# Turning gathered rows with VectorE, in squares of 32, in the down phases of a mixture-of-experts kernel

## The chip, the core and the metric

The kernel runs on one core of a Trainium2 chip. The core has TensorE (PE in the profile, with its weight loads as PEld), VectorE (DVE), ScalarE (ACT), GpSimd (POOL) and SyncE (SP); each works through a queue of its own in order, and they wait for each other by semaphores. The metric is the time of one execution in device microseconds, and the median of three is given.

## What is computed

Three layers follow each other: windowed attention, a gated dense layer, and a mixture of eight experts with two chosen per row. The change lies in the last one.

```python
def _moe2_ref(x, w_gate, w_noise, noise, w1, w2):        # x (2304, 512), w1 (8, 512, 1024), w2 (8, 1024, 512)
    ...                                                 # the two best experts of each row and their weights
    for e in range(E):
        for k in range(2):
            mask = top2[:, k] == e
            ...
            h = np.maximum(x[mask] @ w1[e], 0.0)
            out[mask] += top2_w[mask, k, None] * (h @ w2[e])
```

## The kernel before

**Tiles.** Each expert is given five tiles of 128 rows (`TILES` = 5; `HEAD` = 3 tiles make the first part, `LATE` = 2 the second). GpSimd gathers the 128 rows of tile n from memory into one of two buffers, `x_g[:, n % 2]`, by an indirect DMA (`gather`, L588). The rows lie across the partitions then, and the up product wants the 512 columns across them, in four blocks of 128, so each tile is turned: TensorE does it in `turn_g(n)` (L816), four transposes of 128 x 128 (L822) into one bank, `ps_xt`. ScalarE's `xt_high(n)` (L1066) rounds the turned tile to the format of the products, VectorE's `xt_low(n)` (L1364) takes the remainder; the two halves stand in `xT[p]`. Weights are split in the same manner: eight units per expert arrive in four buffers `raw`, ScalarE's `high(e, n)` (L1052) and VectorE's `low(e, n)` (L1350) make the two halves, and SP loads the next unit when `low` has read its buffer (`load_expert`, L421).

**Order of an expert.** `up(e, p, f)` (L825) multiplies part p with block f of w1 (12 matmuls, 384 columns wide for p = 0 and 256 for p = 1) into one of two banks; ScalarE's `relu` and VectorE's `hidden_low` (L1370) empty it into `hT`. Block f may start when `hidden_low` of block f - 2 is done. After 16 blocks comes the down phase: `down(e, a)` (L842) multiplies the hidden rows of tile a with w2 (24 matmuls of 512 columns), ScalarE's `rows_out` (L1087) scales the result, and GpSimd's `scatter` (L591) adds it to the output in memory, by an indirect DMA.

**Where the turning stands.** Nothing schedules this: each engine's order is written out in its own function. In the down phase of expert e, the five tiles of expert e + 1 are turned, one behind each `down(e, a)`. ScalarE's queue reads there: `high(e+1, a)` for a < 4, `rows_out(e, a)`, `xt_high` of the tile; VectorE's: `low(e+1, a)` for a < 4, `xt_low` of the tile. In the next up half the queues read `relu`, `high` of a unit of w2, and `hidden_low`, `low` of it, for the first four blocks. The first 15 tiles are turned at other places: 0 to 9 in the end of the dense layer and in expert 0, tile 10 behind the last down of expert 0, 11 and 12 inside the second up half of expert 1, 13 and 14 behind its first two downs. `gather(n)` waits until tile n - 2 has been turned (`xt_turned`), and its place in GpSimd's queue is behind `scatter(n - 7)` from tile 17 on.

The index e runs from 0 to 7 everywhere; the last expert's down phase turns nothing. Rows beyond the five tiles of an expert are handled by `left_tile` in a loop that runs as often as such tiles are left.

Of the kernel before, what the change touches and what calls it, by code (L numbers as in the profile page):

```python
# [13 lines left out]
P = 128  # L14


def attention_two_moe_program(nc, q, k, v, gv, w_out, r_gate, r_noise, noise, w1, w2, out):
# [12 lines left out]
    KC = DM // P  # L30
# [31 lines left out]
    PER = TT  # L62
    COLS = NE * PER
# [11 lines left out]
    with ExitStack() as ctx:  # L75
# [64 lines left out]
        more_i = sb("more_i", [P, 3, MORE], I32)  # L140
        idx_r = sb("idx_r", [P, 1], I32)
# [160 lines left out]
        ORDER = [0, 1, 2, 5, 6, 7, 3, 4, 8, 9] + list(range(AHEAD * TILES, ALL))  # L302

# [203 lines left out]
        def _(pool):  # L507
# [137 lines left out]
            for n in (12, 13, 14):  # L645
                gather(n)
            scatter(5)
            gather(15)
            scatter(6)
            gather(16)  # L650
            for m in (7, 8, 9):
                scatter(m)
            for m in range(AHEAD * TILES, ALL):
                scatter(m)
                if m + 7 < ALL:
                    gather(m + 7)
# [20 lines left out]
        def _(pe):  # L677
# [251 lines left out]
            turn_g(10)  # L929
            for f in range(F2C):  # L930
                up(1, 1, f)
                if f in (2, 5):
                    turn_g(11 + f // 3)
            for a in range(TILES):
                down(1, a)
                if a < 2:
                    turn_g(13 + a)
            for e in range(AHEAD, NE):
                for p in range(2):
                    for f in range(F2C):  # L940
                        up(e, p, f)
                for a in range(TILES):
                    down(e, a)
                    if e < NE - 1:
                        turn_g(TILES * (e + 1) + a)
# [27 lines left out]
        def _(act):  # L973
# [92 lines left out]
            def xt_high(n):  # L1066
                e, a = divmod(ORDER[n], TILES)
                p, cols = part(a)
                act.wait_ge(xt_turned, n + 1)
                if e:  # L1070
                    act.wait_ge(up_done, F2C * (half_no(e - 1, p) + 1))
                elif p == 0:
                    act.wait_ge(gv_done, LAST - FC + 6)
                else:
                    act.wait_ge(hr_used, LAST)
                act.copy(xT[p][:, 0, :, cols], ps_xt.rearrange("p (k m) -> p k m", k=KC)).then_inc(xt_hi, 1)  # L1076
# [98 lines left out]
            xt_high(10)  # L1175
            for f in range(F2C):
                relu(1, 1, f)
                if f < KC:
                    high(1, KC + f)
                if f in (2, 5):  # L1180
                    xt_high(11 + f // 3)
            for a in range(TILES):
                if a < KC:
                    high(AHEAD, a)
                rows_out(1, a)
                if a < 2:
                    xt_high(13 + a)
# [31 lines left out]
        def _(dve):  # L1219
# [143 lines left out]

            def xt_low(n):  # L1364
                p, cols = part(ORDER[n] % TILES)
                dve.wait_ge(xt_hi, n + 1)
                dve.tensor_tensor(xT[p][:, 1, :, cols], ps_xt.rearrange("p (k m) -> p k m", k=KC),  # L1367
                                  xT[p][:, 0, :, cols].bitcast(F32), ALU.subtract).then_inc(xt_lo, 1)
# [117 lines left out]
            xt_low(10)  # L1486
            for f in range(F2C):
# [3 lines left out]
                if f in (2, 5):  # L1491
                    xt_low(11 + f // 3)
            for a in range(TILES):
                if a < KC:
                    low(AHEAD, a)
                if a < 2:
                    xt_low(13 + a)
            for e in range(AHEAD, NE):
# [5 lines left out]
                for a in range(TILES):  # L1504
                    if e < NE - 1 and a < KC:
                        low(e + 1, a)
# [42 lines left out]
```

## Time and profile before

| | before |
|---|---|
| median of 3 runs (lowest to highest) | 1055.52 us (1055.36 to 1055.85) |
| the profiled execution, its span from first to last instruction | 1058.44 us, 1056.8 us |
| TensorE busy | 1029.5 us, 97% of the span |
| VectorE, ScalarE, GpSimd busy | 392.2, 387.8, 234.5 us |
| mean granted clock of TensorE | 0.986 |
| memory traffic | 95.28 MB, 90 GB/s on average |

The profile comes from one execution, which took longer than the median of the runs. Busy time says how long an engine had an instruction in work; matmuls overlap, so a busy TensorE is not one at its peak. The granted clock is the share of 2.4 GHz that the chip allowed TensorE: 1.0 is that, 0.5 is 1.2 GHz.

### The profile page before, as it was taken

The numbers are of one execution on the slowest core, as the hardware profiler recorded it, in microseconds if no ns is written. First come the engines' busy times: TensorE is split into PE (matmuls) and PEld (weight loads), VectorE is DVE, ScalarE is ACT, GpSimd is POOL, SyncE is SP. The second block draws the span as 40 slices with busy tenths as digits, with TensorE's granted clock in tenths as the row PEclk, the third lists the DMA queues.
The fourth block names the chain that finished last, engine by engine and source line by source line (L and its number), as shares of the span: only waits on it lengthen the run. The fifth ranks groups of instructions, "written<-read, shape, count | busy, mean of one in ns | idle before, by whom it ended". The sixth has DMA issues, their size and how long they took to land. (4 is left out here: it accounts for less than half of the span.)

```text
span 1056.8 us, 18749 instructions
## 1 busy us (share of the span) xinstructions
PE 1029.5 (97%) x7455; PEld 940.8 (89%) x7455; DVE 392.2 (37%) x1113; ACT 387.8 (37%) x941; POOL 234.5 (22%) x225
## 2 busy tenths in 40 slices
PE   6999999999999999999999999999999999999994
PEld 5999999999999999999999898799898989898983
DVE  3662343342434334242345434433432424343310
ACT  4553243433424333342344433333333333333310
POOL 2581022021111202111022322211304030312111
PEclk6999999999999999999999999999999999999998
DMA  5662113121211212110224232662616263543312
GB/s 174 205 196 71 31 46 96 52 75 51 81 51 50 62 51 81 51 51 1 100 81 147 69 101 41 184 155 58 163 59 153 88 159 100 140 120 100 60 14 37
DMA packets 48249, 95.28 MB, mean 90 GB/s; under 512 B 9504, under 2 KB 14624, under 8 KB 48160
## 3 DMA queue, kind: packets, MB, share of 16 engines
q1 hardware_dynamic: 35696, 66.22, 19.0%
q0 software_dynamic: 12032, 27.31, 12.7%
q8 instruction: 61, 1.00, 0.4%
q10 hardware_dynamic: 432, 0.52, 0.2%
q14 instruction: 28, 0.23, 0.1%
HBM read 72.35 MB, written 21.68 MB: 89 GB/s over the span
## 5 line engine op out<-in xcount | busy, mean ns | idle before, releaser
L760 PEld LDWEIGHTS bank<-xr,wr 128*128 128x128 f32 x2592 | 326.5, 191 | 9.4 <-issue 0.5
L760 PE MATMUL bank<-xr,wr 128*128 128x256 f32 x2592 | 329.3, 283 | 0.0
L838 PE MATMUL bank<-wr 128*128 128x256 f32 (+1 forms) x1536 | 229.8, 310 | 0.6 <-DVE xr L1373 0.3
L838 PEld LDWEIGHTS bank<-wr 128*128 128x128 f32 x1536 | 226.1, 190 | 1.4 <-DVE wr L1373 0.6
L777 PE MATMUL bank<-wr,hr 128*128 128x512 f32 x648 | 176.5, 407 | 0.0
L1267 DVE SCALAR_TENSOR_TENSOR arena<-arena,bank 128x256 f32<-128x256 f32 x108 | 45.4, 420 | 253.0 <-ACT arena L1015 253.0
L1015 ACT ACTIVATE arena<-bank 128x256 f32<-128x256 f32 x108 | 41.5, 384 | 265.9 <-PE bank L760 265.8
L853 PE MATMUL bank<-wr 128*128 128x512 f32 x576 | 136.3, 393 | 0.0
L777 PEld LDWEIGHTS bank<-wr,hr 128*128 128x128 f32 x648 | 113.7, 188 | 23.2 <-issue 2.2
L853 PEld LDWEIGHTS bank<-wr 128*128 128x128 f32 x576 | 106.6, 188 | 21.5
L601 POOL DMA_INDIRECT out<-arena,tab x34 | 53.4, 1572 | 283.8 <-ACT arena L1094 275.3
L529 POOL TENSOR_TENSOR arena<-arena 128x512 f32<-128x512 f32 (+1 forms) x32 | 32.2, 1006 | 319.3 <-DVE arena L1242 319.3
L853 PE MATMUL bank<-wr,xr 128*128 128x512 f32 x384 | 90.8, 393 | 0.0
L1362 DVE TENSOR_TENSOR wr<-arena,wr 128x1024 fp32r<-128x1024 f32 x64 | 78.1, 1225 | 26.6 <-ACT wr L1064 26.6
L853 PEld LDWEIGHTS bank<-wr,xr 128*128 128x128 f32 x384 | 71.2, 188 | 14.4
L1273 DVE TENSOR_TENSOR hr<-arena,hr 128x256 fp32r<-128x256 f32 x108 | 64.4, 596 | 48.2 <-ACT hr L1022 48.2
L1094 ACT ACTIVATE arena<-bank,tab 128x512 f32<-128x512 f32 x34 | 23.4, 690 | 144.1 <-PE bank L853 144.1
L1367 DVE TENSOR_TENSOR wr<-bank,wr 128x512 fp32r<-128x512 f32 x40 | 27.6, 691 | 127.4 <-ACT wr L1076 127.2
L1064 ACT CAST wr<-arena 128x1024 fp32r<-128x1024 f32 x64 | 66.7, 1047 | 0.0
L1022 ACT CAST hr<-arena 128x256 fp32r<-128x256 f32 x108 | 43.9, 406 | 59.0 <-DVE arena L1267 59.0
L571 POOL DMA_INDIRECT places<-pairs,slot_i x36 | 36.2, 1006 | 115.0 <-DVE pairs L1348 106.7
L1373 DVE SCALAR_TENSOR_TENSOR wr<-bank,wr 128x384 fp32r<-128x384 f32 x64 | 35.7, 557 | 64.8 <-ACT wr L1085 64.7
(121 smaller groups left out, 781.5 us busy)
## 6 DMA issues: line engine op xcount, KB each, us to landing
arena<-moe_w SPq DMA_DIRECT2D x64, 512.0 KB, 4.4
arena<-gv SPq DMA_DIRECT2D x12, 512.0 KB, 3.8
out<-zeros POOLq DMA_DIRECT2D x20, 256.0 KB, 2.7
arena<-v SPq DMA_DIRECT2D x18, 256.0 KB, 2.7
x_rows<-arena SPq DMA_DIRECT2D x9, 512.0 KB, 3.1
arena<-v SPq DMA_DIRECT2D x34, 128.0 KB, 2.7
arena<-k SPq DMA_DIRECT2D x17, 256.0 KB, 3.5
arena<-q SPq DMA_DIRECT2D x16, 256.0 KB, 3.6
```

The costliest lines, as they stand in the source:

```text
L571: pool.indirect_dma_start(places[:, :], bass.IndirectOffsetOnAxis(slot_i[:, t, c:c + 1], 0), pairs[:, t, c], None).then_inc(placed if g < ...
L601: pool.indirect_dma_start(out[:, :], bass.IndirectOffsetOnAxis(row_no(m), 0), y_s[:, m % 2], None, compute_op=ALU.add).then_inc(scattered[ ...
L760: mm = pe.matmul(o, gv_w[:, f, w, kk], xr[:, g % 2, x, kk], start=(m + kk + n == 0), stop=(kk == KC - 1 and n == 2), skip_group_check=True)
L777: mm = pe.matmul(ps_y[t], hr[:, f % 2, a, t * P:(t + 1) * P], wo_w[:, b, f], start=(f == 0 and n == 0), stop=(f == FC - 1 and n == 2))
L838: mm = pe.matmul(ps_h[u % 2][:, 0:n], w1_r[e % 2][:, a, kk, f * P:(f + 1) * P], xT[p][:, b, kk], start=(kk + x == 0), stop=(kk == KC - 1 a ...
L853: mm = pe.matmul(ps_e[m % 2], hT[p][:, i, f, cols], w2_r[:, j, f], start=(f + x == 0), stop=(f == F2C - 1 and x == 2))
L1015: act.activation(gate[:, r], ps_g[r][:, 0:GT], ACT.Tanh, scale=0.5).then_inc(gate_done, 1)
L1022: act.copy(hr[:, r, 0], gate[:, r]).then_inc(h_hi, 1)
L1064: act.copy(unit(e, n, 0), raw[:, n % 4]).then_inc(e_hi, 1)
L1267: dve.scalar_tensor_tensor(out=gate[:, r], in0=gate[:, r], scalar=1.0, in1=ps_g[r][:, GT:2 * GT], op0=ALU.add, op1=ALU.mult).then_inc(h_do ...
L1273: dve.tensor_tensor(hr[:, r, 1], gate[:, r], hr[:, r, 0].bitcast(F32), ALU.subtract).then_inc(h_lo, 1)
L1362: dve.tensor_tensor(unit(e, n, 1), raw[:, n % 4], unit(e, n, 0).bitcast(F32), ALU.subtract).then_inc(e_lo, 1)
```

## The change

From tile 10 on (`SQUARES` = `AHEAD * TILES`), TensorE turns no tile. VectorE does it in `turn_rows(n)`: 16 transposes of a square of 32 x 32 in each of the four column blocks, so of 32 partitions by 128 elements, from `x_g` into a new tensor `x_t` of 128 x 4 x 128 in on-chip memory. `xt_high` and `xt_low` read `x_t` in place of the bank (`turned_at`). `turn_rows` waits for the gather, and for `xt_high` and `xt_low` of the tile before, since `x_t` is single. It stands at the head of each tile's work in VectorE's queue in the down phase. The tiles of expert 2 (10 to 14) move into expert 1's down phase, as those of the later experts are in the phase before theirs, and GpSimd's gathers from tile 12 on all stand behind a scatter.

```diff
+    SQUARES = AHEAD * TILES
+    Q4 = P // 4
...
+        x_t = sb("x_t", [P, KC, P])
...
+        def turned_at(n):
+
+            return ps_xt.rearrange("p (k m) -> p k m", k=KC) if n < SQUARES else x_t[:]
...
@@ gpsimd
-            for n in (12, 13, 14):
-                gather(n)
-            scatter(5)
-            gather(15)
-            scatter(6)
-            gather(16)
-            for m in (7, 8, 9):
-                scatter(m)
-            for m in range(AHEAD * TILES, ALL):
+            for m in range(TILES, ALL):
                 scatter(m)
                 if m + 7 < ALL:
                     gather(m + 7)
@@ tensor
             down(0, 4)
-            turn_g(10)
             for f in range(F2C):
                 up(1, 1, f)
-                if f in (2, 5):
-                    turn_g(11 + f // 3)
             for a in range(TILES):
                 down(1, a)
-                if a < 2:
-                    turn_g(13 + a)
...
                 for a in range(TILES):
                     down(e, a)
-                    if e < NE - 1:
-                        turn_g(TILES * (e + 1) + a)
@@ scalar
-                act.copy(xT[p][:, 0, :, cols], ps_xt.rearrange("p (k m) -> p k m", k=KC)).then_inc(xt_hi, 1)
+                act.copy(xT[p][:, 0, :, cols], turned_at(n)).then_inc(xt_hi, 1)
...
             for a in range(TILES):
                 if a < KC:
                     high(AHEAD, a)
                 rows_out(1, a)
-                if a < 2:
-                    xt_high(13 + a)
+                xt_high(SQUARES + a)
@@ vector
+            def turn_rows(n):
+                dve.wait_ge(gathered[n % 2], 16 * (n // 2 + 1))
+                if n > SQUARES:
+                    dve.wait_ge(xt_hi, n)
+                    dve.wait_ge(xt_lo, n)
+                dve.nop(nofuse=True)
+                rows = x_g[:, n % 2].rearrange("p (k m) -> p k m", k=KC)
+                for b in range(4):
+                    at = slice(b * Q4, (b + 1) * Q4)
+                    for a in range(4):
+                        to = slice(a * Q4, (a + 1) * Q4)
+                        tr = dve.transpose(x_t[to, :, at], rows[at, :, to])
+                tr.then_inc(xt_turned, 1)
...
             for a in range(TILES):
+                turn_rows(SQUARES + a)
                 if a < KC:
                     low(AHEAD, a)
-                if a < 2:
-                    xt_low(13 + a)
+                xt_low(SQUARES + a)
...
                 for a in range(TILES):
+                    if e < NE - 1:
+                        turn_rows(TILES * (e + 1) + a)
                     if e < NE - 1 and a < KC:
                         low(e + 1, a)
                     if e < NE - 1:
                         xt_low(TILES * (e + 1) + a)
```

VectorE's queue at the end of a down phase with turning and the start of the next up half, before. L1362 is `low` (behind `up_done` of a w1 unit, behind `down_done` of a w2 unit), L1367 `xt_low`, L1373 `hidden_low`:

```order
L1362 TENSOR_TENSOR wr<-arena,wr 128x1024 [waits up_done,e_hi]
L1367 TENSOR_TENSOR wr<-bank,wr 128x4x128 [waits xt_hi]
L1362 TENSOR_TENSOR wr<-arena,wr 128x1024 [waits up_done,e_hi]
L1367 TENSOR_TENSOR wr<-bank,wr 128x4x128 [waits xt_hi] x2
L1373 SCALAR_TENSOR_TENSOR wr<-bank,wr 128x384 [waits ht_hi]
L1362 TENSOR_TENSOR wr<-arena,wr 128x1024 [waits down_done,e_hi]
```

And the same place in the changed kernel, where L1364 is the squares, L1351 `low`, L1370 `xt_low` and L1376 `hidden_low`:

```order
L1364 STREAM_TRANSPOSE x_t<-arena 32x4x32 [waits xt_lo,gathered0,xt_hi]
L1364 STREAM_TRANSPOSE x_t<-arena 32x4x32 x15
L1351 TENSOR_TENSOR wr<-arena,wr 128x1024 [waits up_done,e_hi]
L1370 TENSOR_TENSOR wr<-x_t,wr 128x4x128 [waits xt_hi]
L1364 STREAM_TRANSPOSE x_t<-arena 32x4x32 [waits xt_lo,gathered1,xt_hi]
L1364 STREAM_TRANSPOSE x_t<-arena 32x4x32 x15
L1370 TENSOR_TENSOR wr<-x_t,wr 128x4x128 [waits xt_hi]
L1376 SCALAR_TENSOR_TENSOR wr<-bank,wr 128x384 [waits ht_hi]
L1351 TENSOR_TENSOR wr<-arena,wr 128x1024 [waits down_done,e_hi]
```

The last two tiles of the phase are shown: 16 squares now stand ahead of each `low` or `xt_low`, and the first hidden row of the next expert stands behind those of the fifth tile.

TensorE's queue between the last tile of a down phase (L853) and the next up half (L838), before and then changed; L822 is the turn:

```order
L853 MATMUL bank<-wr,xr 128x512 [waits ht_lo]
L853 MATMUL bank<-wr,xr 128x512 x2
L822 MATMUL bank<-ident,arena 128x128 [waits gathered1,xt_lo]
L822 MATMUL bank<-ident,arena 128x128 x3
L838 MATMUL bank<-wr 128x384 [waits ht_lo,e_lo,xt_lo]
L838 MATMUL bank<-wr 128x384 x11
L838 MATMUL bank<-wr 128x384 [waits ht_lo]
```

```order
L853 MATMUL bank<-wr,xr 128x512 [waits ht_lo]
L853 MATMUL bank<-wr,xr 128x512 x2
L838 MATMUL bank<-wr 128x384 [waits ht_lo,e_lo,xt_lo]
L838 MATMUL bank<-wr 128x384 x11
L838 MATMUL bank<-wr 128x384 [waits ht_lo]
```

The turn, with its wait for the gather, is gone, and the up half follows the last tile at once.

## Rows read from the trace of the kernel before

**Rows 1.** The page, part 1: busy us, share of the span, instructions.

```profile
PE 1029.5 (97%) x7455; PEld 940.8 (89%) x7455; DVE 392.2 (37%) x1113; ACT 387.8 (37%) x941; POOL 234.5 (22%) x225
```

**Rows 2.** TensorE's waits: who waited for whom, us in total, times, longest.

```profile
PE bank L822 <- DMA arena<-x_rows,tab: 1.7, 1, 1.7
```

**Rows 3.** Timeline, TensorE, down phase of expert 3: start, length, instructions, [idle before].

```profile
783.65 5.64 PE L853 MATMUL bank<-wr 128*128 128x512 f32 x24
...
813.18 28.41 PE L838 MATMUL bank<-wr 128*128 128x384 f32 x192
```

**Rows 4.** Timeline, TensorE, down phase of the last expert.

```profile
1014.75 16.51 PE L853 MATMUL bank<-wr 128*128 128x512 f32 x72
1031.09 11.04 PE L853 MATMUL bank<-wr,xr 128*128 128x512 f32 x48
```

**Rows 5.** Timeline, TensorE, second up half of expert 1.

```profile
654.51 4.55 PE L838 MATMUL bank<-wr 128*128 128x256 f32 x36
...
658.89 0.60 PE L822 MATMUL bank<-ident,arena 128*128 128x128 f32 x4
...
669.49 5.63 PE L853 MATMUL bank<-wr 128*128 128x512 f32 x24
```

**Rows 6.** Timeline, all engines, down phase of expert 2.

```profile
725.87 5.63 PE L853 MATMUL bank<-wr 128*128 128x512 f32 x24
...
726.49 0.42 DVE L1373 SCALAR_TENSOR_TENSOR xr<-bank,xr 128x256 fp32r<-128x256 f32 x1 [1.02 <-ACT xr L1085]
...
737.48 0.69 ACT L1094 ACTIVATE arena<-bank,tab 128x512 f32<-128x512 f32 x1 [3.83 <-PE bank L853]
...
738.93 1.57 POOL L601 DMA_INDIRECT out<-arena,tab  x1 [2.98 <-ACT arena L1094]
739.63 1.23 DVE L1362 TENSOR_TENSOR wr<-arena,wr 128x1024 fp32r<-128x1024 f32 x1 [0.26 <-ACT wr L1064]
740.81 1.01 POOL L588 DMA_INDIRECT arena<-x_rows,tab  x1 [0.30 <-issue]
```

**Rows 7.** Timeline, first blocks of the up half of expert 3.

```profile
755.83 0.58 ACT L1076 CAST wr<-bank 128x512 fp32r<-128x512 f32 x1
756.44 0.69 DVE L1367 TENSOR_TENSOR wr<-bank,wr 128x512 fp32r<-128x512 f32 x1 [5.22 <-ACT wr L1076]
...
757.78 0.49 ACT L1085 ACTIVATE wr<-bank 128x384 fp32r<-128x384 f32 x1 [1.38 <-PE bank L838]
...
758.30 0.56 DVE L1373 SCALAR_TENSOR_TENSOR wr<-bank,wr 128x384 fp32r<-128x384 f32 x1 [1.18 <-ACT wr L1085]
...
759.86 0.49 ACT L1085 ACTIVATE wr<-bank 128x384 fp32r<-128x384 f32 x1 [0.65 <-PE bank L838]
```

**Rows 8.** Timeline, VectorE, attention: masked scores, no wait between.

```profile
12.10 0.29 DVE L1231 CUSTOM_DVE_ANT_0 arena<-bank,mask 128x128 f32<-128x128 f32 x1 [2.45 <-PE bank L706]
...
12.32 0.28 DVE L1231 CUSTOM_DVE_ANT_0 arena<-bank,mask 128x128 f32<-128x128 f32 x1
```

**Rows 9.** Timeline, VectorE: two instructions, the second awaiting the first.

```profile
643.00 0.27 DVE L1467 TENSOR_TENSOR arena<-arena 128x104 f32<-128x104 f32 x1
643.30 0.26 DVE L1468 TENSOR_REDUCE arena<-arena 128x8 f32<-128x104 f32 x1
```

**Rows 10.** DMA issues: count and median us from issue to landing, gathers.

```profile
arena<-x_rows,tab POOLq DMA_INDIRECT x34, 5.1
```

**Rows 11.** Timeline, TensorE, the opening.

```profile
9.80 1.03 PE L724 MATMUL bank<-ident,arena 128*64 128x128 f32 x4 [2.74 <-DVE arena L1248]
```

**Rows 12.** Stretches: busy us of PE, PEld, DVE, ACT, POOL; clock, DMA, GB/s.

```profile
9.00:10.00 1.00, 0.20 (x2) 0.20 (x3) 0.60 (x2) 1.00 (x6) 0.00 (x0) 0.86 1.05 414
...
25.00:26.00 1.00, 1.00 (x22) 0.88 (x22) 0.00 (x0) 0.28 (x2) 0.00 (x0) 0.50 0.98 328
...
30.00:31.00 1.00, 1.00 (x10) 1.00 (x9) 0.00 (x0) 0.00 (x0) 0.00 (x0) 0.90 0.98 318
```

**Rows 13.** The same view, around the wait for tile 12.

```profile
664.00:668.00 4.00, 2.26 (x20) 2.08 (x19) 1.11 (x3) 0.97 (x2) 0.47 (x1) 1.00 0.98 383
```

More of the change, by code:

```diff
@@ L1174, in _ @@
             rows_out(0, 4)
-            xt_high(10)
             for f in range(F2C):
@@ L1179, in _ @@
                     high(1, KC + f)
-                if f in (2, 5):
-                    xt_high(11 + f // 3)
             for a in range(TILES):
@@ L1366, in xt_low @@
                 dve.wait_ge(xt_hi, n + 1)
-                dve.tensor_tensor(xT[p][:, 1, :, cols], ps_xt.rearrange("p (k m) -> p k m", k=KC),
+                dve.tensor_tensor(xT[p][:, 1, :, cols], turned_at(n),
                                   xT[p][:, 0, :, cols].bitcast(F32), ALU.subtract).then_inc(xt_lo, 1)
@@ L1485, in _ @@
             xt_low(9)
-            xt_low(10)
             for f in range(F2C):
@@ L1490, in _ @@
                     low(1, KC + f)
-                if f in (2, 5):
-                    xt_low(11 + f // 3)
             for a in range(TILES):
+                turn_rows(SQUARES + a)
                 if a < KC:
                     low(AHEAD, a)
-                if a < 2:
-                    xt_low(13 + a)
+                xt_low(SQUARES + a)
             for e in range(AHEAD, NE):
```

## The prediction

> **What bounds the kernel now.** I read the page's busy times first. TensorE is busy for 97% of the span and VectorE for 37% [rows 1], so a step that is cut from TensorE's queue shows in the end time, and VectorE has room on average. The waits of TensorE come next: behind the opening, the longest is 1.7 us, the turn of tile 12 waiting for its gathered rows [rows 2]. The end of the kernel is therefore the sum of TensorE's own work. What has to be read after that is one down phase, because the change puts new work on VectorE only there: the average of 37% does not say whether five tiles of turning fit beside five tiles of multiplying.
>
> **What the change removes from TensorE.** 30 turns of four matmuls go: tile 10 behind the first expert, 11 to 14 around the second, and five in each down phase of experts 2 to 6 (numbered from 0). In expert 3 the down phase with its five turns takes 813.18 - 783.65 = 29.53 us [rows 3]. The last expert has no turns: three tiles take 1031.09 - 1014.75 = 16.34 us, 5.45 us each and 27.24 for five [rows 4]. So 2.29 us go per down phase, 0.46 per turn, and 5 x 2.29 = 11.5 us for experts 2 to 6. In expert 1, the second up half holds turns 11 and 12 and the 1.7 us wait. It takes 669.49 - 654.51 = 14.98 us; 36 of its matmuls take 658.89 - 654.51 = 4.38 us, so 96 take 11.68 [rows 5]. That is 3.3 us. Turns 10, 13 and 14 add 3 x 0.46 = 1.4. In all **16.2 us** are taken off TensorE. The last expert's tiles follow each other without a gap, so I expect none between the tiles where the turns stood.
>
> **What it adds on VectorE.** 16 square instructions per tile, each 32 partitions by 128 elements, 480 in all. No row shows a square, nor an instruction that reads or writes other partitions than the one before it. I bound the time from one start to the next by two kinds of rows. Instructions that may overlap: one of 128 elements and its accumulator read start again after 0.21 us, though the first is 0.29 us long [rows 8]. Instructions that each await the one before: 104 elements, start to start 0.30 us, 0.27 us long [rows 9]; 24 more elements at about 1 ns make 0.29 us of length and 0.32 from start to start. So a tile costs between 16 x 0.21 = 3.4 us and 16 x 0.32 = 5.2 us. I take **0.31 us and 4.96 us per tile**. The reason is where they start: in the overlapping rows one instruction follows another on the same 128 lanes, while each square writes another group of 32 partitions than the last (and every fourth reads another), so I place it nearer to the rows that run one after the other; 0.31 is the length of such an instruction with a little of the gap.
>
> The Trainium skill has a rule on this (VectorE: DVE Perf Modes, section on two Vector instructions with no wait between them): an instruction that starts in another quadrant of 32 partitions than the last read or write of that memory is held until all earlier ones have finished. By it all 16 squares are held, which is against this change, and no row here shows it. The same page's section on the three transpose paths gives 311 ns for 128 x 128 elements of 2 bytes; an estimate with it is 16 x 0.311 = 4.98 us per tile, and the total would be the same as mine, while squares that overlapped would make the whole change free, as below.
>
> **Whether that fits.** I count from the start of a down phase, where TensorE would start tiles at 0, 5.45, 10.9, 16.3, 21.8 and the next up half at 27.24. VectorE is free at 1.1: its last hidden row starts 0.62 after the phase and is 0.42 long [rows 6]. Its queue is now, per tile, squares, then the low part of a weight unit (1.23 us) [rows 6], then the low part of the tile (0.69) [rows 7], with 0.1 of overlap and as much of semaphores, 1.9 us in all. The squares of the next tile wait for that last one, because x_t is a single buffer. So the fifth tile is turned at 1.1 + 5 x 4.96 + 4 x 1.9 = 33.5. ScalarE's high part (0.58), VectorE's low part (0.69) and then VectorE's first hidden row of the next expert (0.56) [rows 7] stand behind it in both queues, with some 0.1 of semaphores: 35.5. TensorE may start the third block of the up half only after that hidden row, since the two banks alternate. It would be there at 27.24 + 2 x 2.08 = 31.4 (blocks go by in 2.08 us: 759.86 - 757.78 [rows 7]). **TensorE waits 4.1 us.** There are six such phases (experts 1 to 6), so 24.6 us. The first blocks of the up half need tile 3 of 5 turned (about 20.5) and the fourth weight unit's low part (1.1 + 4 x 4.96 + 3 x 1.9 + 1.2 = 27.9), 0.6 late, which lies inside the same wait. After the third block VectorE needs 0.56 + 1.23 = 1.8 us per block against 2.08, so the delay isn't repeated.
>
> **What else moves.** GpSimd gathers tile n+2 behind the scatter of one tile of the same phase. A scatter starts 1.5 us and a gather 3.3 us after ScalarE starts that tile's output [rows 6], and a gather lands 5.1 us after its issue [rows 10]: 3.0 us after the next tile ends. The squares would start for it at the earliest at that point or, by the chain above, later, so it costs nothing at 4.96 us per tile; and at 3.4 us per tile the 1 us it adds is within the room there. ScalarE now waits with the high part of a tile for the squares, and the next output of rows stands behind that: the first four tiles are turned at 6.1, 12.9, 19.8 and 26.7, the outputs behind them are due at 10.9, 16.3, 21.8 and 27.24, so outputs and scatters keep their times and TensorE finds its banks free. The high part reads on-chip memory in place of a bank; 0.1 us more would add 0.6 to the total. SP's loads of units 4 to 7 wait for the low parts of units 0 to 3; the last is asked for at 27.9 and needed by ScalarE behind the fourth block, after 37, and the nearest landing time, 5.1 us [rows 10], fits. GpSimd's gathers of tiles 12 to 16 now stand behind scatters 5 to 9, as those of the later phases do, and no longer make TensorE wait. What is priced at nothing here would be seen as a wait if the squares were short; behind a wait of 4.1 us it is covered.
>
> **The clock.** A wait of 4 us may cost more than itself. After a wait of 2.74 us of TensorE in the opening, behind sparse work, the clock went from 1.0 to 0.5 (from 2.4 to 1.2 GHz) at about 9.9 us, and came back at about 30, with TensorE busy without a break from 25 on: some 4.5 us [rows 11, 12]. With 1.74 us of wait inside full work it stayed at 1.0 [rows 13]. So each fall costs about half of 4.5, 2.2 us. I count it for three of the six phases, **6.6 us**; bounds 0 and 6 x 2.2 = 13.
>
> **The sum.** -16.2 + 24.6 + 6.6 = +15.0 us. The profiled execution took 1058.44 us (span 1056.8), 2.9 over the median of 1055.52; the median is the one forecast: 1055.5 + 15.0 = **1070.5 us**, and a profile of it some 1073.
>
> **Rivals.**
> A, the squares overlap. At 0.21 us per square a tile costs 3.4 us, the fifth tile is turned at about 28.5 (bounded by TensorE's tiles, no longer by VectorE), the hidden row is ready at 30.4, before 31.4. No wait, the whole gain stays: 1055.5 - 16.2 = 1039.3. For it: VectorE does overlap neighbours in the trace. Against it: the squares change partitions. The point from which it turns is a wait of more than zero at 0.25 us per square, and break-even (16.2 / 6 = 2.7 us of wait) at about 0.29. Chance 0.15.
> B, the squares are a little shorter than I take them, 0.27 to 0.29 us: waits of 1.5 to 2.6 us, no fall of the clock, 1048 to 1056. Each ns per square is 80 ns per phase, half a us on the total. Chance 0.12.
> C, the forecast: 0.30 to 0.325 us, waits of 3.3 to 5.2 us, 1058.9 to 1070.9 without the clock, up to 13 more with it. Chance 0.5.
> D, the squares are longer (a fill of the square before it empties): 0.34 us make 6.4 us of wait per phase and a fall in each: 1055.5 - 16.2 + 38.7 + 13 = 1091. Chance 0.18; of still longer ones, above 1092, 0.05.
>
> **Numbers.** C is the likeliest and gives 1070.5. A range from 1046 to 1092 leaves out A and the very long squares, 2 in 10. Faster by over 0.2% (2.1 us, about what a measurement of this kernel can tell): A and two thirds of B, 0.22. Within 0.2%: 0.04. Slower: 0.74.
>
> **What the profile would show.** The step on TensorE is right if down phases take 27.2 us without a matmul of L822's kind among them. The price is right if squares start 0.31 us apart and the fifth tile's last one ends about 33.5 us after the phase starts. The wait is right if TensorE's longest waits are six of about 4 us on the hidden low rows, at the third block of an up half. Wrong would be: squares 0.2 us apart (A); a wait at the first block instead of the third (the weight unit's low part); or waits on gathered rows.

## The result and the profile after

| | before | changed |
|---|---|---|
| median (lowest to highest) of 4 runs | 1055.65 us (1055.36 to 1055.85) | 1083.01 us (1081.05 to 1084.53) |
| ratio, 95% interval | | 1.0257 (1.0241 to 1.0274) |
| span of the profiled execution | 1056.8 us | 1082.8 us |
| mean granted clock | 0.986 | 0.973 |

The change makes the kernel 27.4 us slower; the two spans differ by 26.0. The page of the changed kernel, busy us, share of the span and instructions, to be held against [rows 1]:

```profile
PE 1029.8 (95%) x7335; PEld 939.7 (87%) x7335; DVE 536.3 (50%) x1593; ACT 389.3 (36%) x941; POOL 243.3 (22%) x225
```

TensorE has 120 transposes less and no less busy time, although they were worth 15 us (experiment 3): something else grew. VectorE went from 392 to 536 us, half of the span. That still looks like an engine with room, and it is the wrong number to look at. TensorE's waits, who waited for whom, us in total, times, longest:

```profile
PE bank L838 <- DVE wr L1376: 19.7, 7, 3.2
PE bank L838 <- issue: 8.0, 6, 1.4
```

There are 27.7 us of waits that [rows 2] did not have, all in the up halves (L838), and the wait for tile 12 is gone. Of the seven waits on L1376 (`hidden_low`) six are 3.2 us long. The six waits called "issue" are the first blocks of the same halves. They can be seen in TensorE's timeline (start, length, instructions, idle before), which answers [rows 3]; this is the down phase of expert 2 and what follows it:

```profile
728.30 16.51 PE L853 MATMUL bank<-wr 128*128 128x512 f32 x72
744.65 11.04 PE L853 MATMUL bank<-wr,xr 128*128 128x512 f32 x48
757.06 4.41 PE L838 MATMUL bank<-wr 128*128 128x384 f32 x24 [1.37 <-issue]
764.71 27.04 PE L838 MATMUL bank<-wr 128*128 128x384 f32 x168 [3.25 <-DVE wr L1376]
791.59 16.51 PE L853 MATMUL bank<-wr 128*128 128x512 f32 x72
```

The five tiles take 27.23 us, as forecast: the second row starts the last two, which take 10.88 us where nothing waits (691.95 - 681.07 in the kernel with one square, experiment 3) and so end at 755.53. The first block of the up half should start there and starts at 757.06, 1.5 late. The third block should start 4.16 later and starts at 764.71, 3.5 late. The last 14 blocks should take 24.1 us (an experiment below shows that length at full clock) and take 791.59 - 764.71 = 26.9. VectorE and ScalarE in that stretch, which answers [rows 6] and [rows 7]:

```profile
755.73 1.23 DVE L1351 TENSOR_TENSOR wr<-arena,wr 128x1024 fp32r<-128x1024 f32 x1
...
757.76 5.05 DVE L1364 STREAM_TRANSPOSE x_t<-arena 32x128 f32<-32x128 f32 x16 [0.20 <-DVE wr L1370]
...
762.85 0.62 ACT L1069 CAST wr<-x_t 128x512 fp32r<-128x512 f32 x1 [5.91 <-DVE x_t L1364]
763.37 0.48 ACT L1078 ACTIVATE wr<-bank 128x384 fp32r<-128x384 f32 x1
763.50 0.69 DVE L1370 TENSOR_TENSOR wr<-x_t,wr 128x512 fp32r<-128x512 f32 x1 [0.68 <-ACT wr L1069]
...
764.11 0.55 DVE L1376 SCALAR_TENSOR_TENSOR wr<-bank,wr 128x384 fp32r<-128x384 f32 x1
```

The first row is the low part of the fourth weight unit, which stands behind the fourth tile's squares. It ends at 756.96, and the first block, which needs it, starts at 757.06; the profile calls that wait "issue". The second row is the fifth tile: 16 squares, starting 0.7 us after TensorE has entered the up half, at 29.5 us of the phase, done at 34.5. Behind it follow without a gap ScalarE's high part (L1069), its `relu` (L1078), VectorE's low part of the tile (L1370) and the hidden row (L1376), and TensorE starts at 764.71 as that ends. The chain of the prediction is there link by link. The clock, one microsecond per row (busy us, instructions, granted clock, DMA, GB/s), around the same wait:

```profile
762.00:763.00 1.00, 0.00 (x0) 1.00 0.51 90
...
764.00:765.00 1.00, 0.29 (x1) 0.50 0.00 0
...
770.00:771.00 1.00, 1.00 (x5) 0.62 0.92 373
```

TensorE works from 764.71 on at 1.2 GHz, until about 770.8: the share of 0.62 is a quarter of that microsecond at full clock. In the first such phase TensorE starts at 702.73 and the clock comes back at 705.9, 3.2 us later:

```profile
705.00:706.00 1.00, 1.00 (x5) 0.55 0.90 172
```

All six lose 1.4 to 2.8 us that way, 11.6 in all: the last 14 blocks take 25.57, 26.88, 25.68, 25.69, 25.50 and 26.87 us.

The account of one execution: waits at the first blocks 6 x 1.5 = 9.0, at the third 6 x 3.5 = 20.9, slow clock 11.6, together 41.5 us; TensorE's saving 15.5 (11.5 in the five later down phases, 4.0 in what stands before them); sum 26.0, which is the difference of the spans.

### The profile page after: what moved, and what is told of

Read it like the earlier page. It is cut to its first block and busy times, and to the rows that moved or that the text cites. A ratio compares the mean times of both kernels' runs of the same rounds, so it can differ in the third digit from the quotient of the medians.

```text
span 1082.8 us, 19018 instructions
## 1 busy us (share of the span) xinstructions
PE 1029.8 (95%) x7335; PEld 939.7 (87%) x7335; DVE 536.3 (50%) x1593; ACT 389.3 (36%) x941; POOL 243.3 (22%) x225
## 5 line engine op out<-in xcount | busy, mean ns | idle before, releaser
L838 PE MATMUL bank<-wr 128*128 128x256 f32 (+1 forms) x1536 | 242.8, 320 | 27.9 <-DVE wr L1376 19.7
L838 PEld LDWEIGHTS bank<-wr 128*128 128x128 f32 x1536 | 237.3, 197 | 33.2 <-DVE wr L1376 21.9
L1364 DVE STREAM_TRANSPOSE x_t<-arena 32x128 f32<-32x128 f32 x480 | 145.3, 303 | 11.0 <-DVE wr L1370 4.9
L853 PE MATMUL bank<-wr 128*128 128x512 f32 x576 | 132.8, 390 | 0.0
L853 PEld LDWEIGHTS bank<-wr 128*128 128x128 f32 x576 | 107.5, 188 | 21.9
L853 PE MATMUL bank<-wr,xr 128*128 128x512 f32 x384 | 88.7, 390 | 0.0
L853 PEld LDWEIGHTS bank<-wr,xr 128*128 128x128 f32 x384 | 71.9, 188 | 14.8
L1351 DVE TENSOR_TENSOR wr<-arena,wr 128x1024 fp32r<-128x1024 f32 x64 | 78.0, 1223 | 12.4 <-ACT wr L1057 11.6
L1376 DVE SCALAR_TENSOR_TENSOR wr<-bank,wr 128x384 fp32r<-128x384 f32 x64 | 35.6, 555 | 59.4 <-ACT wr L1078 59.4
L596 POOL DMA_INDIRECT arena<-x_rows,tab x34 | 43.6, 1283 | 74.2 <-DVE x_t L1364 43.8
```

The costliest lines, as they stand in the source:

```text
L596: pool.indirect_dma_start(x_g[:, n % 2], None, x2_rows[:, :], bass.IndirectOffsetOnAxis(row_no(m), 0)).then_inc(gathered[n % 2], 16)
L838: mm = pe.matmul(ps_h[u % 2][:, 0:n], w1_r[e % 2][:, a, kk, f * P:(f + 1) * P], xT[p][:, b, kk], start=(kk + x == 0), stop=(kk == KC - 1 a ...
L853: mm = pe.matmul(ps_e[m % 2], hT[p][:, i, f, cols], w2_r[:, j, f], start=(f + x == 0), stop=(f == F2C - 1 and x == 2))
L1351: dve.tensor_tensor(unit(e, n, 1), raw[:, n % 4], unit(e, n, 0).bitcast(F32), ALU.subtract).then_inc(e_lo, 1)
L1364: tr = dve.transpose(x_t[to, :, at], rows[at, :, to])
```

## The experiments

Each was timed beside the kernel before on its chip (1056.1 to 1056.7 us there); where two times are compared, the ratios to before are the safer measure.

**1. Are the squares slow because each starts on other partitions?** Every square goes to the partitions it came from, so the rows are not turned across the partitions and the output is wrong:

```diff
-                        tr = dve.transpose(x_t[to, :, at], rows[at, :, to])
+                        tr = dve.transpose(x_t[at, :, to], rows[at, :, to])
```

> As the change, but each square is written to the 32 partitions it was read from, so that 12 of the 16 squares of a tile start on the same partitions as the one before (the rows are then not turned across the partitions, and the output is not the reference's). Theory 1 (a square waits for the end of the one before because it starts on other partitions): the 12 start about 0.21 us apart, the 4 others 0.31; a tile costs about 3.8 us in place of 5.05, the fifth tile is turned before 29.4 us of the phase, no wait of TensorE, 1039 to 1041. Rival (a square costs 0.30 us wherever it lies): starts stay 0.31 to 0.32 us apart and the time stays at 1083.

Measured: 1041.33 us, ratio 0.9855 (0.9839 to 0.9871). VectorE's timeline of one tile, first the changed kernel, then this one:

```profile
729.26 5.04 DVE L1364 STREAM_TRANSPOSE x_t<-arena 32x128 f32<-32x128 f32 x16
```

```profile
721.43 3.57 DVE L1364 STREAM_TRANSPOSE x_t<-arena 32x128 f32<-32x128 f32 x16
```

5.04 against 3.57 us for the same 16 instructions: 0.316 and 0.22 us apart on average. The second average is a mixture, since every fourth square still goes to other partitions than the one before; start by start, averaged over the 30 tiles, the trace has 0.27 us before such a square, 0.23 behind it and 0.19 between the others. The instructions themselves are shorter too (count, then duration in ns, lowest, median and highest; first and last start), again the changed kernel and then this one:

```profile
L1364 DVE STREAM_TRANSPOSE x_t<-arena x480: 291/303/311, 667.3 to 1011.7; 32x128 f32<-32x128 f32 x160
```

```profile
L1364 DVE STREAM_TRANSPOSE x_t<-arena x480: 256/260/309, 665.7 to 971.0; 32x128 f32<-32x128 f32 x160
```

So both bounds of the prediction exist on the chip, 0.31 for squares that change partitions and 0.19 to 0.23 for those that don't, and rival A's time is about what the second would give. That VectorE finishes one square before it starts the next, when the next stands on other partitions, fits the rule of the Trainium skill (VectorE: DVE Perf Modes, section on two Vector instructions with no wait between them): the trace agrees, 0.303 us long and 0.316 apart. (The prediction counted all 16 squares of a tile under that rule; it is 15, since the first stands on the same partitions as the low part before it and waits for that by a semaphore.)

**2. Which change counts, that of the partitions read or written?** The two loops are swapped:

```diff
-                for b in range(4):
-                    at = slice(b * Q4, (b + 1) * Q4)
-                    for a in range(4):
-                        to = slice(a * Q4, (a + 1) * Q4)
+                for a in range(4):
+                    to = slice(a * Q4, (a + 1) * Q4)
+                    for b in range(4):
+                        at = slice(b * Q4, (b + 1) * Q4)
```

> As the change with the two loops over the squares swapped: now the partitions that are read change with each square and those that are written with every fourth. Theory 1 (either change makes the square wait for the end of the one before): starts stay 0.31 us apart, 1083. Rival (only a change of the written partitions does): 12 of 16 squares start 0.21 us apart, no waits, 1041.

Measured: 1082.42 us, ratio 1.025 (1.0233 to 1.0267), a tile in 5.04 us as before. Either change holds a square back, and no order of the 16 avoids both.

**3. What is TensorE's part worth alone, and how does the loss depend on the number of squares?** Two kernels leave squares out from the second turned tile on, 15 of 16 and 2 of 16:

```diff
-                for b in range(4):
+                for b in range(4 if n == SQUARES else 1):
...
-                    for a in range(4):
+                    for a in range(4 if n == SQUARES else 1):
```

```diff
-                    for a in range(4):
+                    for a in range(4 if b < 2 or n == SQUARES else 3):
```

> As the change, but from the second turned tile on only one of the 16 squares is made (15 are left out, the tile is mostly stale, the output is not the reference's). It measures what TensorE's part of the change is worth by itself. Theory: VectorE's queue has room, no waits, 16.2 us less than before: 1039.4 to 1041. Rival (the turns were covered by something else, or a gap opens in their place): 1045 or more.

> As the change, but two of the 16 squares of each tile are left out from the second turned tile on (those parts of the tile are stale, the output is not the reference's). Theory (the queue of VectorE in the down phase sets the end of the phase): a tile costs 14 x 0.316 = 4.42 us, the fifth tile is turned 5 x 0.63 = 3.2 us earlier, the 4.9 us of wait per phase become 1.7 to 1.9, and with so short a wait the clock does not fall: 1039.4 + 6 x 1.8 = 1050, at most 1052. Rival (the time comes from something that does not depend on the number of squares, as the gathered rows or the single x_t): 1078 or more.

Measured: with one square 1041.24 us, ratio 0.9862 (0.9847 to 0.9877), 15.5 us less than before (14.6 by the ratio), so the forecast saving of 16.2 was 0.7 or more too high. With 14 squares 1057.82 us, ratio 1.0011 (1.0001 to 1.0021): two squares in sixteen are worth 1083.0 - 1057.8 = 25 of the 1083.0 - 1041.2 = 42 us that all of them cost. This is 6 to 8 us more than the theory said. TensorE's timeline of the first three up halves with 14 squares (from the third block on, and the down phase behind it) shows a part of why:

```profile
698.90 25.85 PE L838 MATMUL bank<-wr 128*128 128x384 f32 x168 [2.60 <-DVE wr L1376]
724.59 16.51 PE L853 MATMUL bank<-wr 128*128 128x512 f32 x72
...
758.10 24.29 PE L838 MATMUL bank<-wr 128*128 128x384 f32 x168 [1.93 <-DVE wr L1376]
782.23 16.51 PE L853 MATMUL bank<-wr 128*128 128x512 f32 x72
...
815.74 25.85 PE L838 MATMUL bank<-wr 128*128 128x384 f32 x168 [1.93 <-DVE wr L1376]
841.43 16.51 PE L853 MATMUL bank<-wr 128*128 128x512 f32 x72
```

The waits are 1.93 us as forecast, 2.6 in the first phase. But the 14 blocks behind them take 25.7, 24.1 and 25.7 us: the clock fell in the first and the third phase all the same, after waits that short. The three later phases have waits of 1.9 us and no fall. By the trace, the two falls cost 3.2 us; from the first block to the third pass 6.28 us in five phases and 7.01 in the first, against 4.16 when nothing waits, 13.5 us in all where 10.8 were counted; and the kernel without waits takes 1041.2 and not 1039.4. That makes 7.7 us.

**4. Is the rest the clock?** TensorE is given 14 matmuls of zeros to do in the wait (the trace has two instructions for each, 28 in all, 3.29 us):

```diff
                         up(e, p, f)
+                        if p == 0 and f == 1:
+                            for n in range(14):
+                                pe.matmul(ps_xt[:, n % 4 * P:(n % 4 + 1) * P], zeros[:], zeros[:], start=True, stop=True)
```

> As the change, with 14 matmuls of zeros more (128 columns, some 3.1 us at full clock) in TensorE's queue between the second and the third block of each first up half from expert 2 on, into the bank that is idle there; nothing reads them. Theory (the up halves behind the wait are 1.5 to 3 us too long because the clock fell in the wait): TensorE has no long idle time, the clock stays at 1.0, the wait itself is hidden in the added work, and the kernel gets faster by about 12 us: 1070 to 1072. Rival (the halves are long for another reason, a backlog of VectorE or the banks): 1083, or up to 19 us slower if the added matmuls are not covered.

Measured: 1072.32 us, ratio 1.0149 (1.0132 to 1.0166): 84 added matmuls (14 in each of six phases) make the kernel 10.7 us faster, 11.4 by the ratios. Its mean clock is 0.986, that of the kernel before. TensorE's timeline:

```profile
693.98 4.42 PE L838 MATMUL bank<-wr 128*128 128x384 f32 x24 [1.30 <-issue]
698.24 3.29 PE L939 MATMUL bank<-zeros 128*128 128x128 f32 x28
701.63 24.27 PE L838 MATMUL bank<-wr 128*128 128x384 f32 x168
725.73 9.48 PE L853 MATMUL bank<-wr 128*128 128x512 f32 x41
```

From the first block to the third it is 7.65 us, exactly as in the changed kernel (764.71 - 757.06), so VectorE's chain is untouched; behind it 14 blocks take 24.10 us in place of 25.5 to 26.9, in all six phases. Counted from the same place in both traces (the last tiles of expert 0, at 641.73 and 640.62) to the end, the difference is 11.6 us, which is the whole of the slow clock in the account above.

**5. Is the chain through VectorE's queue what the prediction says?** Two kernels move its links. In one the weight unit's low part stands before the squares:

```diff
-                turn_rows(SQUARES + a)
                 if a < KC:
                     low(AHEAD, a)
+                turn_rows(SQUARES + a)
                 xt_low(SQUARES + a)
...                                               # and the same in the loop of the later experts
```

> As the change, but VectorE makes the low part of the weight unit before the squares of the tile, not behind them. Theory 1 (what counts is the chain squares, high part, low part of the tile; the unit's low part hides the high part now): the first block no longer waits, but each of the first four tiles costs about 0.7 us more, so the fifth tile is turned about 3 us later: 1083 + 18 = about 1100. Rival (the late low part of the fourth unit, which holds the first block back by 1.3 us, is a cost of its own): 1083 - 8 = 1075.

Measured: 1103.64 us, ratio 1.0442 (1.0424 to 1.046). Two successive tiles on VectorE:

```profile
733.78 5.04 DVE L1364 STREAM_TRANSPOSE x_t<-arena 32x128 f32<-32x128 f32 x16
739.51 0.69 DVE L1370 TENSOR_TENSOR wr<-x_t,wr 128x512 fp32r<-128x512 f32 x1 [0.69 <-ACT wr L1069]
740.46 1.23 DVE L1351 TENSOR_TENSOR wr<-arena,wr 128x1024 fp32r<-128x1024 f32 x1 [0.26 <-ACT wr L1057]
741.60 5.04 DVE L1364 STREAM_TRANSPOSE x_t<-arena 32x128 f32<-32x128 f32 x16
```

A tile now takes 7.82 us in place of 7.11, 0.69 of it idle before L1370: the high part of the tile, which the weight unit's low part hid, stands open. The wait at the first block is gone and the one at the third is 8.15 us. So the late weight unit was not a cost of its own.

In the other, the turned tile has two buffers:

```diff
+        x_ts = [x_t[:], arena[:, at_y:at_y + DM].rearrange("p (k m) -> p k m", k=KC)]
...
-                if n > SQUARES:
-                    dve.wait_ge(xt_hi, n)
-                    dve.wait_ge(xt_lo, n)
+                if n > SQUARES + 1:
+                    dve.wait_ge(xt_hi, n - 1)
+                    dve.wait_ge(xt_lo, n - 1)
...                                               # x_ts[n % 2] wherever x_t stood
```

> As the change, with a second buffer for the turned tile (in a part of the arena that is idle by then), so that the squares of a tile wait for the high and low part of the tile before the last, not of the last. Theory (VectorE works in order anyway, and only the gap between a tile's low part and the next squares goes): four gaps of 0.2 us per phase, 0.8 us less wait, 5 to 6 us less in all: 1077 to 1079. Rival (the single buffer is what holds VectorE back): a large part of the 28 us of waits goes, 1060 or less.

Measured: 1071.22 us, ratio 1.0134 (1.0117 to 1.0151), 12 us better (13 by the ratios) where 5 to 6 were expected. The squares start before the low part ends, where they started 0.20 us behind it: 0.3 us per tile and not 0.2, so 1.2 us less wait in each phase, 7.3 in all. And the clock fell in four phases and not in six, which gives back 5.2 us; together 12.5, the difference of the two spans. TensorE's timeline of the second and third phase (line numbers of the up half shift by one, L839):

```profile
762.40 24.27 PE L839 MATMUL bank<-wr 128*128 128x384 f32 x168 [2.95 <-DVE wr L1377]
786.51 16.51 PE L854 MATMUL bank<-wr 128*128 128x512 f32 x72
...
821.65 25.84 PE L839 MATMUL bank<-wr 128*128 128x384 f32 x168 [2.95 <-DVE wr L1377]
847.32 16.51 PE L854 MATMUL bank<-wr 128*128 128x512 f32 x72
```

Behind the same wait of 2.95 us the 14 blocks take 24.1 us once and 25.7 us the other time.

**6. Is it the last tile?** TensorE turns the fifth tile of each phase again:

```diff
                 for a in range(TILES):
                     down(e, a)
+                if e < NE - 1:
+                    turn_g(TILES * (e + 2) - 1)
...
-                    if e < NE - 1:
+                    if e < NE - 1 and a < TILES - 1:
                         turn_rows(TILES * (e + 1) + a)
...                                               # the same for the down phase of expert 1, and turned_at gives the bank for these tiles
```

> As the change, but the fifth tile of each of the six down phases is turned by TensorE in a bank, as before. Theory: nothing stands in front of the first hidden row any more, so the wait at the third block goes; the fourth weight unit's low part (28.7 us into the phase by the measured step of 7.1 us per tile) still holds the first block back by 1.0 to 1.3 us, and each phase has one turn of 0.46 us. 1039.4 + 6 x (0.46 + 1.2) = 1049, clock at 1.0. Rival (all of VectorE's turning delays, not the last tile's): some 4/5 of the loss stays, 1075.

Measured: 1058.22 us, ratio 1.0013 (1.0003 to 1.0023). The wait at the third block is gone, as the theory said, but a new one was overlooked:

```profile
PE bank L822 <- issue: 12.1, 7, 1.9
```

```profile
752.40 0.68 DVE L1373 TENSOR_TENSOR wr<-x_t,wr 128x512 fp32r<-128x512 f32 x1
...
753.19 0.63 PE L822 MATMUL bank<-ident,arena 128*128 128x128 f32 x4 [1.88 <-issue]
...
753.57 21.71 PE L838 MATMUL bank<-wr 128*128 128x384 f32 x136
```

`turn_g` waits for the low part of the tile before it, which protected the one bank when all tiles went through it. That low part (`xt_low`, here L1373) ends at 753.08, and TensorE stands 1.88 us ahead of its turn, more than the 1.2 I had for the weight unit. With the turn, 2.4 us go per phase, 14.6 in six. The expected clock of 1.0 did not come either: in the first of the six phases it fell behind this wait, and the up half takes 29.98 us where the other five take 28.43:

```profile
694.11 29.98 PE L838 MATMUL bank<-wr 128*128 128x384 f32 x192
```

The two together, 16.2 us, bring the time back to before.

**7. Do the squares pay at other places?** The fifth tile's squares stand in fours behind the first four hidden rows of the up half; the weight units that stood there follow behind the next four, and the fourth unit's low part moves one tile forward:

```diff
                         hidden_low(e, p, f)
                         if p == 0 and f < KC:
-                            low(e, KC + f)
+                            turn_rows(TILES * (e + 1) - 1, [f])
+                        if p == 0 and f == KC:
+                            xt_low(TILES * (e + 1) - 1)
+                        if p == 0 and f >= KC:
+                            low(e, f)
-                for a in range(TILES):
+                for a in range(TILES - 1):
                     if e < NE - 1:
                         turn_rows(TILES * (e + 1) + a)
-                    if e < NE - 1 and a < KC:
-                        low(e + 1, a)
-                    if e < NE - 1:
+                        for n in units_at[a]:             # (0,), (1,), (2, 3), ()
+                            low(e + 1, n)
                         xt_low(TILES * (e + 1) + a)
...
```

(`turn_rows` takes as its second argument which fourths of the squares to make. ScalarE's queue follows in the same manner.)

> As the change, with the same 480 squares at other places: the fifth tile's 16 squares stand in fours behind the first four hidden rows of the up half, the four weight units that stood there move behind the next four, and the fourth unit's low part moves one tile forward, to the third. Theory (the squares fit if no more than four tiles stand in the down phase and VectorE's 2.08 us per block aren't exceeded): no wait of TensorE over 0.3 us, clock at 1.0, all 30 turns saved: 1039 to 1042, 16 us less than before. Rival (squares disturb wherever they stand, or the blocks of 0.56 + 1.26 us of VectorE are too full): over 1050.

Measured: 1044.02 us, ratio 0.9884 (0.9868 to 0.9901), and on another chip 1044.61, 0.9893 (0.9876 to 0.991). All 480 squares are made, nothing is left out, and it takes 12 us less than before, 2 us more than the expectation allowed. What is left to the 1041.2 of the kernel with one square is in each up half:

```profile
748.08 19.70 PE L838 MATMUL bank<-wr 128*128 128x384 f32 x120
768.02 8.90 PE L838 MATMUL bank<-wr 128*128 128x256 f32 x72 [0.24 <-DVE xr L1383]
776.75 16.51 PE L853 MATMUL bank<-wr 128*128 128x512 f32 x72
```

28.67 us in place of 28.2: VectorE is so full that a hidden row of the second half waits for the last weight unit (that unit's low part runs from 766.40 to 767.63, the hidden row starts at 767.55, and TensorE behind it at 768.02). The unit was moved behind the second block of the second half, beside a repeat of the first version:

```diff
-                        if p == 0 and f >= KC:
-                            low(e, f)
+                        if (p == 0 and KC <= f < F2C - 1) or (p == 1 and f == 1):
+                            low(e, f if p == 0 else F2C - 1)
```

> As e7_spread, but the last weight unit of an expert is split behind the second block of the second up half, no longer behind the last of the first. Theory (what e7_spread still loses, 0.24 us of wait at the third block of the second half and as much of clock-free delay before it, comes from that unit's 1.23 us standing in front of a hidden row): the up half goes from 28.67 to 28.2 us, 0.45 x 6 = 2.7 us less than e7_spread, 1041 to 1042, 15 us less than before. Rival (the rest is from the squares in the first half): no change, 1044.

> e7_spread again, beside e11_last_unit_later on one chip: 1044 by its first measurement.

Measured: 1043.97 us, ratio 0.9884 (0.9868 to 0.9901): no better than the version it was to mend. The half goes from 28.67 to 28.55 us only, since the 1.23 us of the unit now delay the hidden row behind it, in a half where blocks follow each other in 1.44.

**8. Are the phases independent?** Squares for expert 2's tiles alone; TensorE turns the later tiles as before:

```diff
-            return ps_xt.rearrange("p (k m) -> p k m", k=KC) if n < SQUARES else x_t[:]
+            return ps_xt.rearrange("p (k m) -> p k m", k=KC) if n // TILES != AHEAD else x_t[:]
...
                 for a in range(TILES):
                     down(e, a)
+                    if e < NE - 1:
+                        turn_g(TILES * (e + 1) + a)
...                                               # turn_rows goes from VectorE's loop of the later experts
```

> The change in one phase alone: squares for the five tiles of expert 2 in the down phase of expert 1, all later tiles turned by TensorE as before. Theory (the phases are independent): the turns 10 to 14 and the wait for tile 12 are saved, 4.7 us, one phase's waits and slow clock are paid, 4.9 us + 1.5 to 3: 1.7 to 3.2 us more than before. Rival (a delayed phase is partly made up in the next): 0 or less than before.

Measured: 1060.63 us, ratio 1.0038 (1.0024 to 1.0052), 2.5 to 5.5 us more than before. TensorE's timeline has the forecast pieces:

```profile
665.93 16.51 PE L853 MATMUL bank<-wr 128*128 128x512 f32 x72
...
694.62 4.40 PE L838 MATMUL bank<-wr 128*128 128x384 f32 x24 [1.30 <-issue]
702.27 25.86 PE L838 MATMUL bank<-wr 128*128 128x384 f32 x168 [3.25 <-DVE wr L1378]
727.97 5.63 PE L853 MATMUL bank<-wr 128*128 128x512 f32 x24
...
757.49 28.42 PE L838 MATMUL bank<-wr 128*128 128x384 f32 x192
```

Waits of 1.5 and 3.5 us, a half with 1.6 us of slow clock, then the old pace of 29.52 us per down phase (757.49 - 727.97, [rows 3] has 29.53). The pieces add up to 1.5 + 3.5 + 1.6 - 4.0 (the turns and the wait saved) = 2.6 us, and so much the two traces differ from the last tiles of expert 0 on (at 641.25 here, 641.77 before) to the end. That is inside the expectation; the timed difference of 3.9 is somewhat above it, and these few us are at the limit of what the runs tell. Nothing is made up in the next phase.

## Why the prediction was right, and where it was short

The direction and its reason were right, and the time lay in the range; the forecast of 1070.5 us was 12.5 too low: the kernel lost 27.4 us where 15.0 were forecast. The range of 46 us was wide, three times that forecast change, so that the time fell into it says less than the steps do:

- **TensorE's saving**, 16.2 us: 15.5 (experiment 3; the same in the account of the trace). The down phases gave what was forecast. The second up half of expert 1 did not: without its turns and its wait it was to take 11.68 us, by its first three blocks, and takes 666.39 - 654.12 = 12.27. In its middle TensorE waits for VectorE, which has 0.42 us of hidden row and 1.23 of a weight unit to do per block of 1.44:

```profile
654.12 12.44 PE L838 MATMUL bank<-wr 128*128 128x256 f32 x96
666.39 16.51 PE L853 MATMUL bank<-wr 128*128 128x512 f32 x72
```

- **The price of a square**, 0.31 us: 0.316. (The upper bound, 16 x 0.32, is 5.1 us per tile and not 5.2.) The choice between the two bounds decided the sign, and it was right for the reason given: experiment 1 has the other bound, with the other sign.
- **A tile in VectorE's queue**, 4.96 + 1.9 = 6.86 us: 7.11. The squares cost 0.1 more, and behind each low part 0.20 us pass before the next squares, where I had counted some 0.1 of semaphores in all. The fifth tile was turned at 34.5 us, not 33.5. That one microsecond is what the next term was short of.
- **The wait of TensorE**, 4.1 us in each phase, at the third block: 5.0, of it 1.5 at the first block (forecast 0.6, and rightly said to lie inside the same chain, experiment 5) and 3.5 at the third. In all 29.9 for 24.6: +5.3 us. This is the first of two terms with the wrong size.
- **The clock**, three falls of 2.2 us, 6.6 us: all six phases lost 1.4 to 2.8, 11.6 in all: +5.0 us. This is the second. The mechanism was right, and experiment 4 shows it by itself; what failed was taking three of six. The trace of before had a fall after a wait of 2.74 us and none after 1.74, and the waits forecast were over 4. The price of a fall, 2.2 us from the opening, lies between the 1.4 to 1.6 and the 2.8 seen. That it was all six is partly chance: the kernel with the loops swapped has the same waits, and in its profiled execution five phases fell.
- **What was priced at nothing** stayed there: the gathers, the weight loads, the outputs and scatters show no wait of TensorE.
- **Rivals.** A's mechanism does not occur when the squares really turn a tile; its time, 1039.3, was seen at 1041.3 in experiment 1. B's range of 1048 to 1056 was just missed by the kernel with 14 squares (1057.8), whose tile costs as much as one with 16 squares of 0.277 us; its "no fall of the clock" did not hold, since two of six phases fell. By the prediction's own 80 ns for each ns, B's shortest wait should also have been 0.9 us and not 1.5. C came, at 0.316 us and waits of 5.0. D's price per square did not come, but its other half did, a fall of the clock in each phase.

The two short terms are 5.3 + 5.0, and TensorE's saving 0.7: 11.0 us, the whole of what the forecast (+15.0) lacked to the 26.0 of the spans. The timed medians differ by 1.4 more.

## What to carry to other kernels

An engine that is 37% busy can still set the pace of one stage: lay its queue out for that stage, instruction by instruction, and look which of its results the bound engine needs next. Work taken off the bound engine pays only if the last link of the new chain, here the fifth tile, does not stand in front of something that is due; the same 480 squares cost 27 us in one order and gain 12 in another. And a wait of TensorE costs more than its length: add to it what the granted clock may lose behind it, here 1.4 to 2.8 us in most phases.

## What was not expected of the hardware

- A square that writes or reads other partitions than the one before is not only held back, it is longer as well: 303 ns against 260 for the same 32 x 128 elements on the same partitions. In experiment 1 the squares that go to other partitions than the one before are 301 to 307 ns long too. The prediction had a single length.
- The granted clock fell to 1.2 GHz after waits of 1.88 us (first phase of experiment 6) and 1.93 us (third phase with 14 squares), and stayed up after others of 1.93 us in that same execution, of 2.95 us (two buffers) and of 3.24 us (first phase with the loops swapped, rows below). It fell in 1 of 6 phases with waits of 1.9 us before a turn, in 2 of 6 with waits of 1.9 to 2.6 us, 4 of 6 with 2.95, 5 of 6 and 6 of 6 with 3.25, and 6 of 6 with 8.15. Behind the changed kernel's waits it stayed low for 3.2 us in one phase and 6.1 in another. So longer waits had more falls, but the length of the wait alone does not decide it; what does is left open.

```profile
701.30 24.26 PE L838 MATMUL bank<-wr 128*128 128x384 f32 x168 [3.24 <-DVE wr L1376]
725.39 16.51 PE L853 MATMUL bank<-wr 128*128 128x512 f32 x72
```

- Squares that wait for a semaphore of the instruction just before them (the low part) start 0.20 us after its end. In the kernel with two buffers, where they wait for an older low part, they start 0.09 us before it: 734.40 + 0.69 = 735.09 against 735.00. The wait for the neighbour costs 0.3 us (rows below, the kernel with two buffers; the changed kernel's rows show `[0.20 <-DVE wr L1370]`).

```profile
734.40 0.69 DVE L1371 TENSOR_TENSOR wr<-arena,wr 128x512 fp32r<-128x512 f32 x1
735.00 2.18 DVE L1365 STREAM_TRANSPOSE x_t<-arena 32x128 f32<-32x128 f32 x7
```
